# Three chained stages on one core: expert outputs transposed and kept on chip, final MLP run in expert order

## The chip, the cores and the metric

The kernel runs on one core of one Trainium2 chip. The metric is device time in microseconds (us), the median of three runs. One profiled execution of the kernel before is read alongside.

## The reference, cut to what matters

```python
# 1. attention: q, k, v [4, 8, 576, 64]; heads 0-3 see 32 keys back, heads 4-7 every 4th of 128 back
attn = softmax(where(mask, q @ k.T / 8, -1e9));  x = attn @ v          # -> [2304, 512]
# 2. mixture of experts, one of 8 per token
e_idx  = argmax(x @ w_gate)                                            # [2304]
gate_w = softmax(x @ w_gate)[e_idx];  eom = sigmoid(x @ w_output_gate)
out[e_idx == e] = gate_w * eom[:, e] * (relu(x[e_idx == e] @ w1[e]) @ w2[e])   # w1 [8,512,1024], w2 [8,1024,512]
# 3. MLP
result = softplus(out @ w_in) @ w_out                                  # w_in [512,2048], w_out [2048,512]
```

Everything is float32. With the reference's own inputs the eight experts get 370, 280, 356, 312, 196, 203, 278 and 309 tokens.

## The kernel before, in words

All three stages run in one program. TensorE (PE) multiplies float32 data in the fp32r form, each operand split into a high and a low part, so that every product is three matmuls: high by high, low by high, high by low.

**Attention** runs in a loop of two turns of two batches. At its end the token rows are stored to DRAM (`x_tokens`) by the ACT queue, and the gate logits are kept.

**Routing** is one chain of small VectorE (DVE) operations, L950 to L1040, each waiting for the last (`step`). It finds each token's expert and its place in a padded order of slots of 384 rows: slots 0 to 7 belong to experts 0 to 7, and up to five overflow slots take what an expert has over 384. The inverse of that order (`source_i`, which token stands in which row) is made with one-hot matrices: `place_onehot` (a token's place in its block of 128; ACT makes 13 of the 18 token tiles, L777 and L780, DVE the rest) and `block_token` (L999, L1001, with float32 inputs), multiplied in 18 matmuls (L545). At the same time POOL makes the low parts of the first three expert weight chunks (L406).

**Experts.** `Fori(0, E)` over slots. POOL gathers the rows of the next slot with three indirect DMAs (L384), PE transposes them (L554, L562), ACT and DVE split them to `x_hi` and `x_lo`. The hidden size 1024 is cut in eight chunks. For each chunk `f`, `product1` is 12 matmuls whose moving width is the slot's size, and `product2` is 3 matmuls per tile of 128 tokens, 512 columns wide, with the tokens as the stationary side. The slot's size is the smallest of `SIZES = (384, 320, 288, 256)` that holds its tokens (slot 0 always takes 384). PE's program has one unrolled body for each size and picks it by nested `If`s in `sized_slot`. The weights of the next chunks come in a ring of four (`raw`, 512 KB a chunk); ACT writes `w_hi` (L770) and DVE `w_lo` (L1046). The results go over `y_sb` to DRAM (`y_sorted`). Then a loop over the five overflow slots (L642, L643) is walked, whose body (again all four sizes) is jumped over if the slot is not used. Here no slot is.

**Between experts and MLP** all engines meet (`experts_over`), and POOL gathers the first 384 rows from `y_sorted` back in token order (L435). DVE scales them, PE transposes them (L554), ACT and DVE split them.

**MLP.** Six groups of 384 tokens, 16 chunks each: 12 matmuls of 384 columns and 9 of 512. Twelve chunks of weights were split and kept during the experts (`m_hi`, `m_lo`, by POOL), four are split in the first group. The rows of the next group are gathered, scaled and transposed inside each group (12 transposes, L562). Results leave over `y_sb` and the SP queue (L315).

Of the kernel before, what the change touches and what calls it, by code (L numbers as in the profile page):

```python
# [41 lines left out]
SIZES = (SLOT, 320, 288, 256)  # L42
OVER = (N - SLOT) // SLOT
XROWS = (E + OVER) * SLOT
BLOCKS = (E + OVER + 1) * TPS
# [4 lines left out]
RING = 4  # L50
AHEAD = RING - 1
KEPT = FC2 - RING
SCALE = 1.0 / float(np.sqrt(D))
# [5 lines left out]
PLACES_ACT = 13  # L59
# [7 lines left out]
def build(nc, qT, kT, vw, wg, we, wm, out):  # L67
    assert OVER == 5 and NT * P == N and GROUPS * SLOT == N
    ctx = ExitStack()
    with ctx:  # L70
# [8 lines left out]
        ys_d = nc.dram_tensor("y_sorted", (XROWS, DM), F32).ap()  # L79
# [4 lines left out]
        dest_i = sb(ctx, "dest_i", [P, NT], I32)  # L84
        source_i = sb(ctx, "source_i", [P, BLOCKS], I32)
        scale_t = sb(ctx, "scale_t", [P, NT])
        flags_i = sb(ctx, "flags_i", [1, OVER + 1], I32)
        taken_i = sb(ctx, "taken_i", [1, E + OVER], I32)
        raw = sb(ctx, "raw", [P, RING, WCOLS])
        w_hi = sb(ctx, "w_hi", [P, RING, WCOLS], F32R)  # L90
        w_lo = sb(ctx, "w_lo", [P, RING, WCOLS], F32R)

# [5 lines left out]
        v_sb = [sb(early, f"v_sb{s}", [P, UNITS, H, D]) for s in range(2)]  # L98
        x_sb = sb(early, "x_sb", [P, NT, DM])
# [7 lines left out]
        emin8 = sb(early, "emin8", [P, E])  # L107
        thresholds = sb(early, "thresholds", [P, OVER])
        slot_no = sb(early, "slot_no", [P, OVER])
        not_first = sb(early, "not_first", [P, E, NT])  # L110
        column_no = sb(early, "column_no", [P, P])
        block_row = sb(early, "block_row", [P, BLOCKS])
        token_no = sb(early, "token_no", [P, NT])
        logits_01 = sb(early, "logits_01", [P, NT, 2, 2 * E])
        logits_23 = sb(early, "logits_23", [P, NT, 2 * E])
        with ExitStack() as attn:
            probs = sb(attn, "probs", [QT, BANKS, HEADS, KEYS])
# [6 lines left out]
        route = {n: sb(early, f"route_{n}", [P, NT]) for n in  # L124
                 ("m", "first", "sum", "z", "ez", "den", "r", "b1", "b2", "over", "dest", "place", "block")}
# [7 lines left out]
        ov = sb(early, "ov", [P, E])  # L133
        ov_cum = sb(early, "ov_cum", [P, E])
        base2 = sb(early, "base2", [P, E])
        fl = sb(early, "fl", [P, OVER + 1])
        fl_cmp = sb(early, "fl_cmp", [P, OVER, E])
        taken = sb(early, "taken", [P, E + OVER])
        rank_i = sb(early, "rank_i", [P, NT], I32)
        place_onehot = sb(early, "place_onehot", [P, NT, P], F16)  # L140
        in_block = sb(early, "in_block", [P, NT, BLOCKS])
        block_token = sb(early, "block_token", [P, NT, BLOCKS], F16)
# [3 lines left out]

        xs_sb = sb(ctx, "xs_sb", [P, TPS, DM])
        x_hi = sb(ctx, "x_hi", [P, KC, SLOT], F32R)
        x_lo = sb(ctx, "x_lo", [P, KC, SLOT], F32R)
        h_hi = sb(ctx, "h_hi", [P, RING, SLOT], F32R)  # L150
        h_lo = sb(ctx, "h_lo", [P, RING, SLOT], F32R)
        y_sb = sb(ctx, "y_sb", [P, TPS, DM])
        yg_sb = sb(ctx, "yg_sb", [P, TPS, DM])
        soft = sb(ctx, "soft", [P, 2, SLOT])
        g_sb = sb(ctx, "g_sb", [P, 2, SLOT])
        raw_m = sb(ctx, "raw_m", [P, WCOLS])
        m_hi = sb(ctx, "m_hi", [P, KEPT, WCOLS], F32R)
        m_lo = sb(ctx, "m_lo", [P, KEPT, WCOLS], F32R)

# [8 lines left out]
        m_h_ps = [bank[0], bank[1], bank[3]]  # L168
        t_ps = [bank[2], bank[3], bank[7], bank[2]]
        first_t_ps = t_ps[0:3] + [bank[6]]  # L170
# [9 lines left out]
        zero_filled = sem("zero_filled")  # L180
# [8 lines left out]
            exp_in_ready, exps_gate_done, dest_ready, route_done, x_stored, place_ready, place_distances, place_onehots, \  # L189
            block_tokens, sources_summed, sources_ready = map(sem, (  # L190
                "tile_done", "x_copied_act", "x_copied_dve", "route_step",
                "onehot_ready", "ranks_done", "exp_in_ready", "exps_gate_done", "dest_ready", "route_done",
                "x_stored", "place_ready", "place_distances", "place_onehots", "block_tokens", "sources_summed", "sources_ready"))
        raw_loaded = [sem(f"raw_loaded{r}") for r in range(RING)]
        first_rows = [sem(f"first_rows{j}") for j in range(TPS)]
        first_gathered = [sem(f"first_gathered{j}") for j in range(TPS)]
        w_hi_done, w_lo_done = sem("w_hi_done"), sem("w_lo_done")
        rows_loaded, rows_t_done, x_hi_done, x_lo_done = map(sem, (
            "rows_loaded", "rows_t_done", "x_hi_done", "x_lo_done"))
        g1_done, g2_done, h_hi_done, h_lo_done, y_copied, y_stored, y_all_stored = map(sem, (  # L200
            "g1_done", "g2_done", "h_hi_done", "h_lo_done", "y_copied", "y_stored", "y_all_stored"))
        mraw_loaded, m_hi_done, m_lo_done = sem("mraw_loaded"), sem("m_hi_done"), sem("m_lo_done")
        experts_over, overflow_stored = sem("experts_over"), sem("overflow_stored")
        tail_loaded = [sem(f"tail_loaded{r}") for r in range(RING)]
        tail_hi_done, tail_lo_done = sem("tail_hi_done"), sem("tail_lo_done")
        gathered, rows_scaled, m_rows_t_done, m_x_hi_done, m_x_lo_done = map(sem, (
            "gathered", "rows_scaled", "m_rows_t_done", "m_x_hi_done", "m_x_lo_done"))
# [5 lines left out]
        SCORE_CREDIT, PT_CREDIT, OUT_CREDIT, TILE_CREDIT, PLACE_CREDIT, W_CREDIT, H_CREDIT, G_CREDIT, G2_CREDIT, Y_CREDIT = \  # L213
            BANKS, 1, 2, 2, 1, RING, 2, 3, 1, 1
# [937 lines left out]
```

## Time and profile before

| what | value |
|---|---|
| median of 3 runs (lowest, highest) | 855.58 us (854.88, 857.57) |
| profiled execution, span | 854.7 us, 0.9 us under the median |
| PE busy | 788.7 us, 92% |
| DVE busy | 426.5 us, 50% |
| ACT busy | 400.4 us, 47% |
| POOL busy | 142.7 us, 17% |
| attention | 0 to 136.6 us |
| routing, up to the first expert matmul | to 165.2 us |
| experts | to 417.8 us |
| between experts and MLP | to 438.7 us |
| MLP, up to its last copy | to 849.7 us |

Busy time is an average over stages. PE is busy nearly all the time in attention, experts and MLP; it is nearly idle in the routing and between experts and MLP. A matmul's start to start, not its duration, tells its price, since matmuls overlap.

### The profile page before, as it was taken

To read this page: it belongs to the slowest core of one execution; us is meant where nothing else is said; L and a number is where in the kernel's file an instruction comes from. 1 tells how busy PE (TensorE), PEld (TensorE's weight loads), DVE (VectorE), ACT (ScalarE), POOL (GpSimd) and SP (SyncE) were. 2 spreads that over 40 slices of the span, in tenths; PEclk is the share of its full clock that TensorE was granted. 3 is DMA by queue.
4 is the path that set the end of the run, shared out by engine and by line. 5 is a ranking of instruction groups with operands and counts; after the bars stand their busy time and mean duration, and the time that the engine had idled before them with its cause. 6 is when DMAs were issued, how large, how long until landed. Compare 5 with 4: busy or idle time off the path is not lost.

```text
span 854.7 us, 13304 instructions
## 1 busy us (share of the span) xinstructions
PE 788.7 (92%) x4472; PEld 688.2 (81%) x4473; DVE 426.5 (50%) x856; ACT 400.4 (47%) x1015; POOL 142.7 (17%) x139
## 2 busy tenths in 40 slices
PE   5998993498999999999569999999999999999997
PEld 3676673497899998889459999989999999999996
DVE  7886977543644466655134434443434434434332
ACT  4885983333445456544134344334335335335332
POOL 4220223322331332514120100100100100000000
PEclk9999997599999999999859999999999999999999
DMA  9568905245464677754140100100100100000000
GB/s 258 151 186 289 247 5 184 78 144 199 151 219 142 237 258 249 238 201 172 40 173 0 38 23 15 37 0 37 37 0 37 35 2 37 0 0 37 1 1 38
DMA packets 35796, 89.66 MB, mean 105 GB/s; under 512 B 3824, under 2 KB 12016, under 8 KB 35248
## 3 DMA queue, kind: packets, MB, share of 16 engines
q1 hardware_dynamic: 28032, 66.36, 24.1%
q0 software_dynamic: 5328, 18.09, 6.7%
q10 hardware_dynamic: 2400, 4.72, 1.5%
q8 instruction: 23, 0.38, 0.2%
q14 instruction: 13, 0.11, 0.0%
HBM read 69.50 MB, written 19.66 MB: 104 GB/s over the span
## 4 chain that ended last, share of the span: by engine, by line
PE 79%; PEld 6%; DVE 4%; issue 4%; DMA 2%; ACT 2%; PEldq 2%; SPq 1%; POOL 0%; ACTq 0%; DVEq 0%; POOLq 0%
PE bank L573 11%; PE bank L575 11%; PE bank L574 11%; PE bank L584 11%; PE bank L586 11%; PE bank L582 11%; PE bank L460 4%; PE bank L484 2%; PE bank L497 2%; PE bank L470 2%; PE bank L562 1%; DMA v_sb<-vw 1%; PEld bank L573 1%; PEld bank L575 1%; PEld bank L586 1%
## 5 line engine op out<-in xcount | busy, mean ns | idle before, releaser
L1095 DVE SCALAR_TENSOR_TENSOR g_sb<-bank,soft 128x384 f32<-128x384 f32 x96 | 53.6, 558 | 229.4 <-ACT soft L846 229.4
L842 ACT ACTIVATE soft<-bank 128x384 f32<-128x384 f32 x96 | 47.3, 492 | 209.6 <-PE bank L575 209.6
L1046 DVE TENSOR_TENSOR w_lo<-raw,w_hi 128x1024 fp32r<-128x1024 f32 x65 | 89.3, 1373 | 78.8 <-ACT w_hi L770 77.8
L573 PE MATMUL bank<-x_hi,w_hi 128*128 128x384 f32 (+3 forms) x352 | 112.2, 319 | 5.3 <-issue 3.7
L575 PE MATMUL bank<-x_hi,w_lo 128*128 128x384 f32 (+3 forms) x352 | 111.9, 318 | 0.6 <-issue 0.6
L574 PE MATMUL bank<-x_lo,w_hi 128*128 128x384 f32 (+3 forms) x352 | 111.7, 317 | 0.0
L770 ACT ACTIVATE w_hi<-raw 128x1024 fp32r<-128x1024 f32 x68 | 71.8, 1058 | 77.1 <-PE bank L586 75.5
L582 PE MATMUL bank<-w_hi,h_hi 128*128 128x512 f32 x248 | 99.6, 402 | 0.5 <-DVE h_lo L1059 0.5
L573 PE MATMUL bank<-x_hi,m_hi 128*128 128x384 f32 x288 | 98.2, 341 | 0.6 <-DVE x_lo L1053 0.6
L575 PE MATMUL bank<-x_hi,m_lo 128*128 128x384 f32 x288 | 98.1, 341 | 0.0
L574 PE MATMUL bank<-x_lo,m_hi 128*128 128x384 f32 x288 | 97.8, 339 | 0.0
L586 PE MATMUL bank<-w_hi,h_lo 128*128 128x512 f32 x248 | 97.5, 393 | 0.0
L584 PE MATMUL bank<-w_lo,h_hi 128*128 128x512 f32 x248 | 97.4, 393 | 0.0
L586 PE MATMUL bank<-m_hi,h_lo 128*128 128x512 f32 x216 | 85.5, 396 | 0.0
L584 PE MATMUL bank<-m_lo,h_hi 128*128 128x512 f32 x216 | 85.3, 395 | 0.0
L582 PE MATMUL bank<-m_hi,h_hi 128*128 128x512 f32 x216 | 84.0, 389 | 0.0
L710 ACT ACTIVATE probs<-bank,neg_max 96x128 f32<-96x128 f32 x192 | 67.3, 364 | 23.1 <-DVE neg_max L881 23.1
L573 PEld LDWEIGHTS bank<-x_hi,w_hi 128*128 128x128 f32 x352 | 67.4, 192 | 10.2 <-issue 4.6
L574 PEld LDWEIGHTS bank<-x_lo,w_hi 128*128 128x128 f32 x352 | 67.4, 191 | 3.2
L575 PEld LDWEIGHTS bank<-x_hi,w_lo 128*128 128x128 f32 x352 | 67.4, 191 | 0.0
L435 POOL DMA_INDIRECT yg_sb<-y_sorted,dest_i x18 | 18.5, 1029 | 254.8 <-DVE xs_sb L1084 226.3
L573 PEld LDWEIGHTS bank<-x_hi,m_hi 128*128 128x128 f32 x288 | 55.1, 191 | 3.6 <-DVE x_lo L1053 1.0
(147 smaller groups left out, 1347.9 us busy)
## 6 DMA issues: line engine op xcount, KB each, us to landing
raw<-we SPq DMA_DIRECT2D x64, 512.0 KB, 3.9
raw_m<-wm POOLq DMA_DIRECT2D x12, 512.0 KB, 8.1
y_sorted<-y_sb SPq DMA_DIRECT2D x24, 256.0 KB, 5.3
x_tokens<-x_sb ACTq DMA_DIRECT2D x6, 768.0 KB, 5.8
out<-y_sb SPq DMA_DIRECT2D x18, 256.0 KB, 2.1
v_sb<-vw SPq DMA_DIRECT2D x4, 1024.0 KB, 12.0
y_sorted<-k_sb SPq DMA_DIRECT2D x1, 3840.0 KB, 31.0
q_sb<-qT SPq DMA_DIRECT2D x4, 768.0 KB, 8.1
```

Source lines behind the costliest of these rows:

```text
L460: last = nc.tensor.matmul(bank_[0:QT, 2 * KEYS * n_pair:2 * KEYS * (n_pair + 1)], q_sb[b][:, pair, q0:q0 + QT], k_sb[b][:, pair, :, k0:k0 ...
L573: nc.tensor.matmul(bank_[:, 0:rows], hi[:, w], x_hi[:, k, 0:rows], start=(k == 0), stop=False)
L574: nc.tensor.matmul(bank_[:, 0:rows], hi[:, w], x_lo[:, k, 0:rows], start=False, stop=False)
L575: last = nc.tensor.matmul(bank_[:, 0:rows], lo[:, w], x_hi[:, k, 0:rows], start=False, stop=(k == KC - 1))
L582: nc.tensor.matmul(y_ps[j][:, :], h_hi[:, f % RING, c], hi[:, DM:2 * DM], start=(f == 0), stop=False, skip_group_check=True)
L584: nc.tensor.matmul(y_ps[j][:, :], h_hi[:, f % RING, c], lo[:, DM:2 * DM], start=False, stop=False, skip_group_check=True)
L586: last = nc.tensor.matmul(y_ps[j][:, :], h_lo[:, f % RING, c], hi[:, DM:2 * DM], start=False, stop=(f == n_f - 1), skip_group_check=True)
L710: last = nc.scalar.activation(probs[:, c, h, :], s_ps[c][0:QT, KEYS * h:KEYS * (h + 1)], ACT.Exp, bias=neg_max[:, c, h:h + 1], scale=SCALE ...
L770: nc.scalar.activation(w_hi[:, r, :], raw[:, r, :], ACT.Copy).then_inc(done, 1)
L842: nc.scalar.activation(u, m_h_ps[f % 3][:, 0:SLOT], ACT.Abs).then_inc(soft_step, 1)
L1046: nc.vector.tensor_tensor(w_lo[:, r, :], raw[:, r, :], w_hi[:, r, :].bitcast(F32), ALU.subtract).then_inc(done, 1)
L1095: nc.vector.scalar_tensor_tensor(g_sb[:, f % 2, :], m_h_ps[f % 3][:, 0:SLOT], 0.0, soft[:, f % 2, :], ALU.max, ALU.add).then_inc(g_done, 1)
```

## The change

- The experts' `product2` is turned round: the weights are the stationary side and the slot's tokens the moving side, so it is 12 matmuls of the slot's size per chunk instead of 3 matmuls of 512 columns per tile. Its result is y transposed, which is copied (four ACT copies) into `yT_sb`, on chip, at the expert's start column. `y_sorted`, its zero fill, the meeting of the engines, the second gather and the MLP's transposes are gone.
- The MLP walks the tokens in expert order; `group_rows_hi` and `group_rows_lo` split straight from `yT_sb`. The results are scattered to `out` by 18 indirect DMAs on POOL, whose row numbers come from `expert_order`, a DRAM table written by 18 indirect DMAs on POOL ahead of the expert loop.
- Each token's scale is stored to DRAM and gathered by three more indirect DMAs per slot; ACT scales the expert's input rows (`scale_rows`) ahead of their transposes.
- `SIZES` gets a fifth entry, 224, and slot 0 takes its real size; the overflow body is one unrolled size (384).
- The one-hots are all made on DVE from 16-bit inputs. DVE also makes the low parts of the first four weight chunks, which POOL no longer does.
- The ring is eight chunks, four split ahead; `w_lo` is written over `raw`. A chunk is loaded once `g2_done` says its place is free. Eight MLP chunks are kept and eight split in the first group.
- Only two PSUM banks hold transposes, so they are done as (0, 1) and (2, 3), with a wait on `x_lo_done` between.

```diff
-SIZES = (SLOT, 320, 288, 256)
+SIZES = (SLOT, 320, 288, 256, 224)
-RING = 4
-AHEAD = RING - 1
+RING = FC1
+AHEAD = 4
...
+                if not slot:
+                    pool.wait_ge(scales_stored, 16)
+                for j in range(TPS):
+                    c = slot * TPS + j
+                    pool.indirect_dma_start(
+                        out=row_scale[:, c:c + 1], out_offset=None, in_=scale_d,
+                        in_offset=bass.IndirectOffsetOnAxis(ap=source_i[:, c:c + 1], axis=0)
+                        ).then_inc(rows_loaded if slot else first_rows[j], 16)
...
-            for f in range(AHEAD):
-                pool.wait_ge(w_hi_done, f + 1 + W_CREDIT)
-                nc.gpsimd.tensor_tensor(w_lo[:, f, :], raw[:, f, :], w_hi[:, f, :].bitcast(F32), ALU.subtract
-                                        ).then_inc(w_lo_done, 1)
...
+            pool.wait_ge(positions_ready, 1)
+            for t in range(NT):
+                pool.indirect_dma_start(
+                    out=order_d, out_offset=bass.IndirectOffsetOnAxis(ap=position_i[:, t:t + 1], axis=0),
+                    in_=token_ids[:, t:t + 1], in_offset=None).then_inc(order_written, 16)
+            pool.wait_ge(order_written, 16 * NT)
+            pool.dma_start(out_rows_i[:, :], order_d.rearrange("(p t) o -> p (t o)", p=P)).then_inc(out_rows_loaded, 16)
...
+            def product2_columns(f, hi, lo, done, rows):
+                for k in range(KC):
+                    w = slice(DM + P * k, DM + P * (k + 1))
+                    y = yT_ps[k][:, 0:rows]
+                    nc.tensor.matmul(y, hi[:, w], h_hi[:, f % HRING, 0:rows], start=(f == 0), stop=False,
+                                     skip_group_check=True)
+                    nc.tensor.matmul(y, lo[:, w], h_hi[:, f % HRING, 0:rows], start=False, stop=False,
+                                     skip_group_check=True)
+                    last = nc.tensor.matmul(y, hi[:, w], h_lo[:, f % HRING, 0:rows], start=False,
+                                            stop=(f == FC1 - 1), skip_group_check=True)
+                last.then_inc(done, 1)
...
                 for f in range(FC1):
                     p1(f)
+                    if f == FC1 - 1:
+
+                        pe.wait_ge(rows_scaled, slot * TPS + 2 * TPS)
+                        transpose_rows((0, 1))
                     if f:
-                        if f == FC1 - 1:
-
-                            pe.wait_ge(rows_loaded, slot * (16 * TPS) + 16 * TPS)
-                            transpose_rows((0, 1, 2), rows_t_done)
                         p2(f - 1)

-                pe.wait_ge(x_lo_done, slot * KC + (KC + 1))
-                transpose_rows((3,), rows_t_done)
+                pe.wait_ge(x_lo_done, slot * KC + (KC + 2))
+                transpose_rows((2, 3))
                 p2(FC1 - 1)
...
                 with pe.If(n < used):
-                    sized_slot(n + E)
-            pe.drain().then_inc(experts_over, 1)
-            pe.wait_ge(experts_over, 5)
+                    slot_products(n + E, SLOT)
...
+                    if f == FC1 - 2:
+
+                        act.wait_ge(rows_loaded, slot * (32 * TPS) + 32 * TPS)
+                        for j in range(TPS):
+                            scale_rows(slot + 1, j)
...
+            V.tensor_tensor(place_onehot[:, :, :], column_no[:, :, :],
+                            place[:, :].unsqueeze(1).to_broadcast([P, P, NT]), ALU.is_equal).then_inc(block_tokens, 1)
+            step(V.tensor_tensor(in_block[:, :, :], block_row[:, :, :],
+                                 block_of[:, :].unsqueeze(1).to_broadcast([P, BLOCKS, NT]), ALU.is_equal))
```

## Rows read from the trace of the kernel before

**Rows 1.** Busy time by stretch: PE, PEld, DVE, ACT, POOL, then PEclk, DMA share, GB/s

```profile
136.60:165.24 28.64, 4.80 (x33) 2.98 (x33) 21.87 (x60) 10.40 (x23) 10.96 (x7) 0.58 0.33 110
165.24:417.80 252.56, 247.19 (x1392) 221.94 (x1392) 132.21 (x159) 118.50 (x178) 81.25 (x60) 0.99 0.57 191
417.80:438.65 20.85, 3.44 (x13) 2.14 (x13) 2.07 (x5) 2.71 (x7) 4.13 (x5) 0.57 0.31 95
438.65:849.68 411.03, 410.99 (x2076) 372.71 (x2076) 164.36 (x330) 169.14 (x330) 14.39 (x14) 0.99 0.07 24
...
165.24:168.30 3.06, 3.06 (x10) 3.06 (x11) 0.80 (x2) 0.00 (x0) 2.45 (x4) 0.51 0.55 146
```

**Rows 2.** Groups by form: first products of the slots of size 256

```profile
L573 PE MATMUL bank<-x_hi,w_hi 128*128 128x256 f32 x64 | 18.2, 284 | 0.5 <-issue 0.5
```

**Rows 3.** Timeline of PE in slots 2 and 5: start, us, instruction

```profile
240.22 0.33 PE L573 MATMUL bank<-x_hi,w_hi 128*128 128x384 f32 x1
...
242.30 0.39 PE L582 MATMUL bank<-w_hi,h_hi 128*128 128x512 f32 x1
...
244.38 0.33 PE L573 MATMUL bank<-x_hi,w_hi 128*128 128x384 f32 x1
...
330.34 0.28 PE L573 MATMUL bank<-x_hi,w_hi 128*128 128x256 f32 x1
...
332.61 0.28 PE L574 MATMUL bank<-x_lo,w_hi 128*128 128x256 f32 x1
```

**Rows 4.** Timeline of PE: first matmul of slots 1 and 5

```profile
204.94 0.39 PE L573 MATMUL bank<-x_hi,w_hi 128*128 128x288 f32 x1 [3.27 <-issue]
...
329.89 0.38 PE L573 MATMUL bank<-x_hi,w_hi 128*128 128x256 f32 x1 [0.46 <-issue]
```

**Rows 5.** Chain that ended last, between experts and MLP: start, us, what

```profile
419.39 7.81 PEldq L643
...
432.69 3.68 DMA yg_sb<-y_sorted,dest_i
```

**Rows 6.** Instruction DMA: whole span, 0:165, 165:240, 414:438, 438:855 (packets, MB, share)

```profile
q8 instruction: 23, 0.38, 0.2%
...
q8 instruction: 4, 0.07, 0.2%
...
q8 instruction: 8, 0.13, 0.7%
...
q8 instruction: 5, 0.08, 2.0%
...
q8 instruction: 6, 0.10, 0.1%
```

**Rows 7.** Timeline of DVE in the routing

```profile
137.94 0.31 DVE L955 TENSOR_TENSOR routee_d<-logits,route_m 128x144 f32<-128x144 f32 x1
...
138.97 2.01 DVE L959 TENSOR_TENSOR onehot_b<-emin,route_first 128x144 bf16<-128x144 f32 x1
...
143.38 2.33 DVE L963 TENSOR_TENSOR routee_tmp<-logits,routee_onehot 128x144 f32<-128x144 f32 x1
...
152.66 0.94 DVE L1001 TENSOR_TENSOR block_token<-in_block,token_no 128x756 f16<-128x756 f32 x1
...
155.53 0.19 DVE L1011 CAST source_i<-source 128x42 int32<-128x42 f32 x1
```

**Rows 8.** Timeline of POOL: weight splits and a row gather

```profile
138.44 7.10 POOL L406 TENSOR_TENSOR w_lo<-raw,w_hi 128x1024 fp32r<-128x1024 f32 x3 [13.69 <-ACT w_hi L770]
...
159.37 0.95 POOL L384 DMA_INDIRECT xs_sb<-x_tokens,source_i  x1 [0.30 <-issue]
```

**Rows 9.** Timeline of ACT at the end of the program

```profile
849.68 1.57 ACT L853 ACTIVATE y_sb<-bank 128x512 f32<-128x512 f32 x3 [4.56 <-PE bank L586]
```

**Rows 10.** Chain that ended last: transposes at the end of an MLP group

```profile
504.45 0.98 PE bank L562 x9
```

**Rows 11.** Groups by line: split of a weight chunk on DVE

```profile
L1046 DVE TENSOR_TENSOR w_lo<-raw,w_hi 128x1024 fp32r<-128x1024 f32 x65 | 89.3, 1373 | 78.8 <-ACT w_hi L770 77.8 <-issue 1.0
```

More of the change, by code:

```diff
@@ L97, in build @@
         k_sb = [sb(early, f"k_sb{s}", [P, PAIRS, 2, S]) for s in range(2)]
-        v_sb = [sb(early, f"v_sb{s}", [P, UNITS, H, D]) for s in range(2)]
-        x_sb = sb(early, "x_sb", [P, NT, DM])
+        x_sb = sb(early, "x_sb", [P, TILES_TURN, DM])
         xT_sb = sb(early, "xT_sb", [P, KC, 2 * S])
@@ L116, in build @@
         with ExitStack() as attn:
+            v_sb = [sb(attn, f"v_sb{s}", [P, UNITS, H, D]) for s in range(2)]
             probs = sb(attn, "probs", [QT, BANKS, HEADS, KEYS])
@@ L124, in build @@
         route = {n: sb(early, f"route_{n}", [P, NT]) for n in
-                 ("m", "first", "sum", "z", "ez", "den", "r", "b1", "b2", "over", "dest", "place", "block")}
+                 ("m", "first", "sum", "z", "ez", "den", "dest", "shift", "position", "index")}
         routee = {n: sb(early, f"routee_{n}", [P, NT, E]) for n in
@@ L142, in build @@
-        block_token = sb(early, "block_token", [P, NT, BLOCKS], F16)
+        per_expert = {n: sb(early, f"expert_{n}", [P, E]) for n in
+                      ("ov", "ov_cum", "before", "row", "counted", "shift", "limit", "end")}
+        per_slot = {n: sb(early, f"slot_{n}", [P, SLOTS]) for n in ("expert", "expert8", "start", "taken")}
+        slot_cmp = sb(early, "slot_cmp", [P, SLOTS, E])
+        slot_tmp = sb(early, "slot_tmp", [P, SLOTS, E])
+        place_i = sb(early, "place_i", [P, NT], I32)
@@ L666, in p2 @@
                     pe.wait_ge(g_lo_done, g * FC2 + (f + 1))
-                    product2(f, FC2, *chunk(f), m_g2_done)
+                    product2_rows(f, *chunk(f), m_g2_done)
                 for f in range(FC2):
@@ L863, in _ @@
         def _(dve):
+            for n in range(2):
+                nc.vector.memset(bank[n][:, 2 * TW:SLOT], 0.0)
             for s in range(2):
@@ new lines, in _ @@
+            step(V.tensor_tensor(X["end"][:, :], count, X["row"][:, :], ALU.add))
+            step(V.tensor_tensor(slot_tmp[:, :, :], slot_cmp[:, :, :], over_slots(X["end"][:, :]), ALU.mult))
+            step(V.reduce_sum(SL["taken"][:, :], slot_tmp[:, :, :], axis=AX.X))
+            step(V.scalar_tensor_tensor(SL["taken"][:, :], slot_no[:, :], float(-SLOT), SL["taken"][:, :],
+                                        ALU.mult, ALU.add))
+            step(V.tensor_scalar(SL["taken"][:, :], SL["taken"][:, :], 0.0, None, ALU.max))
@@ new lines, in _ @@
+            step(V.tensor_copy(used_i[:, :], X["ov_cum"][0:1, E - 1:E]))
+            step(V.tensor_copy(expert_i[:, :], SL["expert"][0:1, :]))
+            step(V.tensor_copy(start_i[:, :], SL["start"][0:1, :]))
+            V.tensor_copy(taken_i[:, :], SL["taken"][0:1, :]).then_inc(route_done, 1)
+            step(V.tensor_tensor(RE["tmp"][:, :, :], RE["onehot"][:, :, :], over_t(X["shift"][:, :]), ALU.mult))
+            step(V.reduce_sum(R["shift"][:, :], RE["tmp"][:, :, :], axis=AX.X))
+            step(V.tensor_tensor(R["position"][:, :], R["dest"][:, :], R["shift"][:, :], ALU.add))
```

502 lines of the change are left out of this document (229 added, 273 removed).

## The prediction

> **What bounds the kernel now.** I read the page first: PE is busy 92% of the span, so only PE's work and PE's idle stretches can move the end. Then I cut the span into stages [rows 1]. In experts and MLP PE is busy for 247.2 of 252.6 us and for 411.0 of 411.0. In the routing it works 4.8 of 28.6 us, and between experts and MLP 3.4 of 20.9. So there are two kinds of gain: fewer matmul columns, and shorter gaps. The reader should see that DVE, ACT and POOL have room in the experts (132, 119 and 81 of 253 us), and that DMA is at 57% there.
>
> The price of a matmul is its start to start. In slot 2, 12 matmuls of 384 columns take 2.08 us and 9 of 512 take 2.08; in slot 5, 19 of 256 take 2.27 [rows 3]. That is 0.173, 0.231 and 0.120 us, or 0.00042 us per column; between them 320 columns cost 0.146 and 288 cost 0.133, and continued, 224 cost 0.106.
>
> The sizes: 256 columns occur 64 times in one of the three forms of `product1`, that is two slots of 32 [rows 2]; 320 and 288 likewise two each, 384 the other two. The token counts give 384, 288, 384, 320, 256, 256, 288, 320, and after the change 224 for slots 4 and 5.
>
> **The matmuls of the experts.** `product2` per chunk goes from 9 x 0.231 = 2.08 (6 x 0.231 = 1.39 at size 256) to 12 times the slot's price: 384: 2.08, no gain; 320: 1.75, so 0.33 x 16 chunks = 5.2 us; 288: 1.60, 0.48 x 16 = 7.7; 224: 1.27, 0.12 x 16 = 1.9. `product1` at 224 saves 12 x 0.0135 x 16 = 2.6. Together -17.3. If 224 columns are no quicker than 256, `product2` there costs 1.43 and the gain is 12; those are the ends.
>
> **The routing.** Three DVE operations with 144 elements take from 138.97 to 145.71 us, 6.7 us, while a fourth of the same size takes 0.31 [rows 7]. They stand under POOL's three weight splits, which run from 138.44 to 145.54 [rows 8]. Without those splits they cost about 3 x 0.34. The rest of the new chain to `source_i`: 15 small operations, 4.2 us by their neighbours; three one-hot operations of 2304, 756 and 756 elements, 2.6 + 0.9 + 0.9 = 4.4 by the 0.94 us row with float32 inputs; PE's 18 small matmuls and two conversions, 1.5. From 138.9 that makes 11.6 us against 16.8 now (to 155.72): -5.2, between -3 and -7.5 (half the price for the 16-bit operations is the lower end; I take the row). The Trainium skill, page "VectorE: DVE Perf Modes", section "Mode 2×_1P", says that two-source operations on 16-bit contiguous data give two results per cycle; no row here shows it, and by it the routing would be another 2 us shorter.
>
> From `source_i` to the first product are 9.5 us now. Three more gathers follow the row gathers on POOL, at 1.3 us each (0.95 and 0.30 of issue [rows 8]); the last starts 6.8 us after `source_i` and lands 3.6 later (a gather on its way takes 3.68 [rows 5]). Then ACT's scaling 0.6 and the 2.2 us that follow a landing today. That is 13.2. DVE arrives at the same time: 21 slot operations, eight position operations, a register load and four splits of 1.23 to 1.37 us [rows 11]. +3.8, between +2.5 and +6.
>
> **Slot 0 waits for slot 1's rows.** POOL's queue now has, before `load_rows(1)`, 18 scatters at 1.3 us, the wait for their landing, a load and a register load; six gathers follow. From `source_i`: 8 + 23.4 + 3 + 1.5 + 6.5, last landing +3.6: 45.5. PE wants the scaled rows after the last `product1` of slot 0, at 13.3 + 1.4 (low clock) + 29.2 = 43.9; ACT needs 1.6 for scaling. So PE stalls 3.2, and the late ACT and DVE work costs about 1.3 more: +4.5, from 0 (gathers of single words quicker) to +7.
>
> **Slot changes.** Before the second transpose pair PE waits for two `x_lo` instead of one, and ACT has the row scaling (1.5 us) and a weight split (1.0) in front of the last `h_hi`. At size 224 a `product` lasts 1.3 us; ACT and DVE reach `x_lo` 1 about 1.15 us late, at 288 about 0.25; two slots each, +2.9 (0 to +6). PE's own branch code shows as "issue": 0.46 us before slot 5 [rows 4]. The 224 body lies one `If` deeper (0.4 us) and the last product is shorter, so three changes show 1 to 1.5 us instead of two with 0.6: +2.0 (1 to 4).
>
> **Code that is not loaded.** Slot 1 starts after 3.27 us of "issue" [rows 4], when PE for the first time jumps over three bodies; the first jumps over the overflow body hold PE's queue for 7.81 us [rows 5]. Instruction blocks of 16 KB explain it: eight come from 165 to 240 us, and as 4 + 8 + 5 + 6 make all 23, none from 240 to 414, where six slots run on what is held [rows 6]. After the change a body has 204 matmuls instead of 180, and there are five: matmuls and their weight loads go from 1392 to 2040. The bodies of 288 and 224 now lie behind ones that never ran, so each first entry should miss once: 3.7 us at slot 1 and 3.7 plus the clock's fall at slot 4. I take +9; from 0 (held or fetched early) to +36 (the first rival).
>
> **Between experts and MLP.** The gap is 20.85 us now [rows 1]. After: four copies of y (1.6), ACT's walk over the overflow loop, x_hi 0.5, x_lo 0.55: 4.4. PE's queue walks the same loop, some 5 us, starting 2 us before the array ends, plus 0 to 3.7 for a jump over a body that is a quarter as long. I take 6.9: -14, from -6.5 (the 7.8 us jump stays) to -17. The low clock at the start remains: ten matmuls in 3.06 us at 0.51 [rows 1].
>
> **MLP and end.** Five groups lose 12 transposes, 9 of which take 0.98 [rows 10]: 1.3 x 5 = -6.5. The splits of `x_hi`, `x_lo` lie under the last two `product2`. At the end ACT's copies start at 849.68 [rows 9] and today all is over at 854.7. POOL's three scatters would start at 850.4, 851.8 and 853.1 and land 3.6 later, and 0.8 follows, as today: 857.5, +2.8 (1.5 to 4). The stores inside the MLP are hidden by a whole group of 68 us.
>
> **Sum.** -17.3 - 5.2 + 3.8 + 4.5 + 2.9 + 2.0 + 9 - 14 - 6.5 + 2.8 = -18.0 against the span of 854.7: 836.7, and the median stands 0.9 higher: 838. Attention keeps its operations; the raw loads move to a time when DMA waits for nobody.
>
> **Rivals.** First, on the other side: the five bodies don't stay loaded. Then each change of slot meets one or two blocks that are gone, 3.7 us each with little cover, and the clock falls after each: over six changes some 5 to 6 us each, +27 over my +9: 865. For it speak the 47% more code and the price of a jump to code that is not held; against it, that 174 us passed without one load [rows 6]. It decides from about 18 us more than my sum. The Trainium skill, page "Runtime: NRT & Kernel Launch", section "Instruction fetch mechanics", gives PE room for 2048 instructions and a stall for a taken branch outside what is held; by it 1392 and a few would fit, as the trace shows, and 2040 and a few would not, which is this rival.
>
> Second: the chain of small waits is worse than I add up. POOL's 18 scatters take 2 us each, ACT becomes late in every slot, the 224 slots run at ACT's and DVE's pace: +12, 850.
>
> Third: the code is held and the overflow jump is short, -9 and -3: 826.
>
> **Chances.** My case 0.45, the first rival 0.25, the second 0.15, the third 0.15. A measurement of this kernel tells about 0.3% (2.6 us) from no change. Faster takes my case, the third and most of the second, and a little of the first: 0.72; same 0.05; slower 0.23. The range 824 to 868 leaves 0.1 on either side. My own case alone spans 829 to 847.
>
> **What would show it.** Right: in the routing, the three 144-element operations at 0.3 us each; PE's "issue" only at slots 1, 4 and 5; slots of 320 near 28 us and of 288 near 26; 5 to 8 us before the MLP; MLP groups of 66.8 us. A wait of PE for scaled rows at the end of slot 0 near 3 us. Wrong: instruction packets spread over all slots, "issue" of 3 us or more at most slot changes, `product2` at 224 columns no quicker than 0.12 us a matmul, or an overflow jump that still holds PE for 12 us.

## The result and the profile after

The changed kernel takes **919.18 us** (median of 4 runs, 916.03 to 919.76), the kernel before 855.23 (852.80 to 857.57): ratio 1.0737, 95% interval 1.0712 to 1.0762. It is 7.4% slower. The forecast was 838 us with a range of 824 to 868 and "faster" at 0.72: wrong in sign and outside the range. The time given below for the kernel called four_both is the median of its three fast executions (828.3 to 829.3 us); its other three took 843.9 to 848.3, and its trace is of the one at 848.3, so that trace can't be set beside this time.

The page of the changed kernel: first the span, then busy time per engine, the clock in 40 slices (tenths of full speed), the instruction DMA (packets, MB, share), the chain, and the costliest group of instructions.

```profile
span 914.3 us, 13460 instructions
...
PE 776.8 (85%) x4640; PEld 701.0 (77%) x4641; DVE 419.5 (46%) x854; ACT 409.5 (45%) x1041; POOL 164.7 (18%) x172
...
PEclk9999995977999978697888999999999999999997
...
q8 instruction: 48, 0.79, 0.4%
...
PE 75%; issue 11%; DVE 5%; POOL 4%; ACT 3%; DMA 0%; ACTq 0%; POOLq 0%; DVEq 0%
...
L557 PE MATMUL bank<-x_hi,w_hi 128*128 128x384 f32 (+3 forms) x448 | 149.8, 334 | 71.0 <-issue 69.9
```

PE waits 69.9 us for nothing that the profile names ("issue"), all of it ahead of one kind of instruction, the first product of a slot, where the kernel before had 3.7. And 48 blocks of instructions are fetched where it was 23 [rows 6].

Busy time by stretch: routing from the same point as before, experts, gap, MLP, end. Two short rows behind them show the products after a stall.

```profile
136.60:159.86 23.26, 5.43 (x33) 3.76 (x33) 20.11 (x66) 6.76 (x12) 9.79 (x8) 0.50 0.17 52
159.86:490.86 331.00, 246.36 (x1632) 243.09 (x1632) 127.55 (x159) 127.14 (x208) 99.81 (x90) 0.86 0.40 133
490.86:495.88 5.02, 0.17 (x3) 0.00 (x1) 0.62 (x2) 2.81 (x7) 0.00 (x0) 0.83 0.40 134
495.88:899.65 403.77, 403.73 (x2016) 366.17 (x2016) 161.50 (x319) 172.43 (x333) 14.52 (x15) 0.99 0.03 10
899.65:914.30 14.65, 0.00 (x0) 0.00 (x0) 0.00 (x0) 1.57 (x3) 2.88 (x3) 0.64 0.14 54
...
328.50:333.75 5.25, 5.25 (x24) 5.25 (x25) 1.41 (x2) 1.44 (x2) 3.40 (x2) 0.50 0.01 3
```

Set against [rows 1] this is the whole account: up to the first product -5.4 us (165.24 to 159.86), experts +78.4 (252.56 to 331.00), gap -15.8 (20.85 to 5.02), MLP -7.3 (411.03 to 403.77), end +9.6 (5.0 to 14.65). The sum is +59.6, the difference of the spans. Everything but the experts and the end went about as forecast. The prediction's signs of being wrong came true: 40 of the 48 instruction packets come in the expert stage, at nearly every slot, and "issue" of 3 us or more at most slot changes. In the experts PE is busy for 246 of 331 us, at a mean clock of 0.86 where it was 0.99.

The timeline of PE, first transpose at the end of slot 0 and first product of slots 1, 2, 4, 5, 6 and 7, with the idle time before each and what ended it:

```profile
199.90 1.54 PE L546 MATMUL bank<-ident,xs_sb 128*128 128x128 f32 x6 [9.14 <-ACT xs_sb L766]
...
216.32 0.60 PE L557 MATMUL bank<-x_hi,w_hi 128*128 128x288 f32 x1 [8.77 <-issue]
...
249.98 0.68 PE L557 MATMUL bank<-x_hi,w_hi 128*128 128x384 f32 x1 [3.79 <-issue]
...
328.50 0.55 PE L557 MATMUL bank<-x_hi,w_hi 128*128 128x224 f32 x1 [9.56 <-issue]
...
377.41 0.55 PE L557 MATMUL bank<-x_hi,w_hi 128*128 128x224 f32 x1 [21.85 <-issue]
...
418.18 0.60 PE L557 MATMUL bank<-x_hi,w_hi 128*128 128x288 f32 x1 [14.24 <-issue]
...
459.52 0.63 PE L557 MATMUL bank<-x_hi,w_hi 128*128 128x320 f32 x1 [11.69 <-issue]
```

Six of seven slot changes stall. Slots 4 and 5 are of the same size and run the same body, and still the change between them is the longest. In the trace's records of PE's sequencer these stalls are branches: a jump takes 0.07 to 0.35 us when all is well, and in the expert stage 15 of them take 2.7 to 6.1 us, 70.9 us together. Ahead of slot 5 they stand in a row (start, us, line):

```
353.62 3.58 L635   end of the loop, back to its start
358.03 5.32 L628   past the body of 384
363.54 5.69 L628   past the body of 320
369.50 2.74 L628   past the body of 288
372.42 4.50 L628   past the body of 256
```

And after these stalls PE starts at the lower of its two clock levels (0.50 granted, 1.2 GHz). After the one of 9.56 us, 24 products of 224 columns took 5.25 us at 0.50 (row 328.50 above), 0.22 us each, where later ones take 0.112; after the one of 3.79 us too, products of 384 columns start 0.32 us apart where later ones start 0.173 apart.

### The profile page after: what moved, and what is told of

It is laid out like the page before. It is cut to its first block, busy times and chain, and to the rows that moved or that the text cites. A ratio compares the mean times of both kernels' runs of the same rounds, so it can differ in the third digit from the quotient of the medians.

```text
span 914.3 us, 13460 instructions
## 1 busy us (share of the span) xinstructions
PE 776.8 (85%) x4640; PEld 701.0 (77%) x4641; DVE 419.5 (46%) x854; ACT 409.5 (45%) x1041; POOL 164.7 (18%) x172
## 4 chain that ended last, share of the span: by engine, by line
PE 75%; issue 11%; DVE 5%; POOL 4%; ACT 3%; DMA 0%; ACTq 0%; POOLq 0%; DVEq 0%
PE bank L557 11%; PE bank L559 11%; PE bank L558 11%; PE bank L580 7%; PE bank L582 7%; PE bank L578 7%; PE bank L445 3%; PE bank L567 3%; PE bank L571 3%; PE bank L569 3%; POOL expert_order L396 2%; PE bank L469 2%; PE bank L482 2%; PE bank L455 2%; PE bank L546 1%
## 5 line engine op out<-in xcount | busy, mean ns | idle before, releaser
L557 PE MATMUL bank<-x_hi,w_hi 128*128 128x384 f32 (+3 forms) x448 | 149.8, 334 | 71.0 <-issue 69.9
L558 PE MATMUL bank<-x_lo,w_hi 128*128 128x384 f32 (+3 forms) x448 | 148.2, 331 | 0.0
L559 PE MATMUL bank<-x_hi,w_lo 128*128 128x384 f32 (+3 forms) x448 | 148.1, 331 | 0.0
L557 PEld LDWEIGHTS bank<-x_hi,w_hi 128*128 128x128 f32 x448 | 90.3, 202 | 74.9 <-issue 71.3
L1059 DVE SCALAR_TENSOR_TENSOR h_lo<-bank,h_hi 128x384 fp32r<-128x384 f32 x64 | 35.6, 557 | 156.8 <-ACT h_hi L783 151.5
L567 PE MATMUL bank<-h_hi,w_hi 128*128 128x384 f32 (+3 forms) x256 | 79.7, 311 | 1.6 <-issue 1.6
L569 PE MATMUL bank<-h_hi,w_lo 128*128 128x384 f32 (+3 forms) x256 | 78.1, 305 | 0.0
L571 PE MATMUL bank<-h_lo,w_hi 128*128 128x384 f32 (+3 forms) x256 | 78.0, 305 | 0.0
L557 PE MATMUL bank<-x_hi,m_hi 128*128 128x384 f32 x192 | 65.7, 342 | 4.9 <-DVE x_lo L1084 4.9
L559 PE MATMUL bank<-x_hi,m_lo 128*128 128x384 f32 x192 | 65.6, 341 | 0.0
L558 PE MATMUL bank<-x_lo,m_hi 128*128 128x384 f32 x192 | 65.3, 340 | 0.0
```

The lines of the kernel that those rows point to most:

```text
L557: nc.tensor.matmul(bank_[:, 0:rows], hi[:, w], x_hi[:, k, 0:rows], start=(k == 0), stop=False)
L558: nc.tensor.matmul(bank_[:, 0:rows], hi[:, w], x_lo[:, k, 0:rows], start=False, stop=False)
L559: last = nc.tensor.matmul(bank_[:, 0:rows], lo[:, w], x_hi[:, k, 0:rows], start=False, stop=(k == KC - 1))
L567: nc.tensor.matmul(y, hi[:, w], h_hi[:, f % HRING, 0:rows], start=(f == 0), stop=False, skip_group_check=True)
L569: nc.tensor.matmul(y, lo[:, w], h_hi[:, f % HRING, 0:rows], start=False, stop=False, skip_group_check=True)
L571: last = nc.tensor.matmul(y, hi[:, w], h_lo[:, f % HRING, 0:rows], start=False, stop=(f == FC1 - 1), skip_group_check=True)
```

## The experiments

All ratios are to the kernel before, timed beside each. Instructions are counted in the built programs; a block is the 16 KB of one instruction fetch, 256 instructions. A slow jump is a branch record of PE's sequencer of 2.7 us or more; "in the loop" leaves out those over the overflow body behind it.

**First four: one body less, two bodies less, and never-run bodies added to the kernel before.**

```diff
 a_no256: -SIZES = (SLOT, 320, 288, 256, 224)
          +SIZES = (SLOT, 320, 288, 224)
 a_three: +SIZES = (SLOT, 320, 224)
 b_dose1 (kernel before), b_dose2 with it twice:
                 from_size(0)
+                with pe.If(taken > N):
+                    slot_products(slot, SLOT)
```

> The changed kernel without the 256-row body. No expert of this input takes it (the loads are 370, 280, 356, 312, 196, 203, 278, 309 rows), so every product that runs is the same; the tensor engine's expert loop is 437 instructions shorter (1,751 in place of 2,188; the kernel before has 1,515). Theory A (the bodies of the expert loop no longer stay loaded): the 15 jumps of 2.7 to 6.1 us, 71 us in all, mostly vanish, and the time is 848 to 865; the instruction packets fall from 48 to under 32. If only some vanish, between 865 and 900. Rival B (the longer chain of branches and value loads costs in itself): only experts 4 and 5 pass one branch less, 1 to 2 us together, so 916 to 919. Rival C (low clock and late rows set the gaps): no change, 919.

> The changed kernel with bodies for 384, 320 and 224 rows alone: 1,314 instructions in the loop, fewer than before. Two experts of 280 and 278 rows now take 320 rows in place of 288: 2 x 192 products x (0.147 - 0.133) us = 5.4 us more. Theory A: no jump over 2 us is left; 916 - 71 + 5.4 plus what the clock gives back (up to 17): 835 to 853. Rival B: 919 + 5.4 - 3 = 921. Rival C: 924.

> The kernel before with one more 384-row body at the end of the expert loop that no expert ever takes (its condition is more rows than there are tokens). The work is unchanged; the loop grows from 1,515 instructions to about 1,900. Theory A, form 1 (what counts is the length of the loop, blocks that are only jumped over too): some stalls, 858 to 890. Theory A, form 2 (only blocks that run count): one more jump per expert that lands in one more block, 855 to 860. Rival B: 8 branches more at 0.3 to 0.5 us, 858.

> The kernel before with two more such bodies that no expert takes: the loop has about 2,290 instructions, more than the changed kernel's 2,188. Theory A, form 1: stalls as in the changed kernel, 15 or more of 3 to 6 us, 890 to 930. Theory A, form 2: two more blocks for the two landings, 856 to 870. Rival B: 16 branches more at 0.3 to 0.5 us, 861.

Measured: a_no256 921.02 us (1.0751, 1.0707 to 1.0796), a_three 864.93 (1.0085, 1.0051 to 1.0119), b_dose1 856.0 (0.9991) and b_dose2 857.4 (1.0005). The last two say nothing of the question: the build knows that `taken` can't pass N and left the bodies out, so these are 21 more executions of the kernel before (their traces show the same 61 branches of PE as its own). The other two are the finding. Taking out 437 of 2,188 instructions of the loop gave nothing: 14 slow jumps remain, and theory A's 848 to 865 was missed by 56 us. Taking out the same again removed 56 us and all slow jumps in the loop but two, though theory A had expected none and 835 to 853. So stalls do not grow evenly with the code, they set in at a limit. Rivals B (branch depth) and C (late rows), which a_no256 alone could not rule out, are out: they expected 921 to 924 for a_three.

A rule that fits, made after these runs: PE holds eight blocks, beside the running block it always takes in the next one, and the one unused for longest goes. Worked through over the paths of the eight experts it gives 1 slow jump in the loop for the kernel before (1 seen), 15 for the changed kernel (15), 13 for a_no256 (14), 1 for a_three (2). The loops touch 7, 10, 8 and 6 blocks. It makes two odd predictions, and the next runs test them.

**Same code, moved by 109 instructions; and a never-run body that the build can't leave out.**

```diff
 a_aligned: SIZES = (SLOT, 320, 288, 224), and
+            for _ in range(218):
+                pe.wait_ge(block_tokens, 2)
             first_transposes()
 b_extra (kernel before):
                 from_size(0)
+                with pe.If(used > 3):
+                    slot_products(slot, SLOT)
```

(The build folds two waits into one instruction.)

> The changed kernel without its 256-row body, with 109 more instructions (waits that are already met) on the tensor engine before the first transposes. The expert loop keeps its 1,751 instructions but now lies in seven pieces of 256 instructions in place of eight. Theory A1 (the engine keeps eight such pieces and always takes the next one beside the one that it runs, the longest unused goes): with that rule the run without the 256-row body should show 13 slow jumps (14 were seen), the one with three bodies 1 (2 were seen), the changed kernel 15 (15 were seen); here it gives 2. So the slow jumps fall from 14 to 2 to 4, and the time from 921 to 850 to 862. Rival A2 (the number of instructions or of bodies counts, not where they lie): 14 slow jumps, 921 to 927. Rival C (late rows, clock): 921 to 927.

> The kernel before with one more 384-row body at the end of the expert loop, under a condition that this input never meets but that the build can't decide (more than three overflow slots); in the two runs with the other condition the build had left the bodies out, so they were repeats of the kernel before. The work is unchanged, the loop has about 1,905 instructions, in nine pieces of 256 of which eight are run or landed in. Theory A1: 21 slow jumps in place of 1, at 3.6 to 6 us each of which the queue in front of the engine hides up to 1: 925 to 960. Rival A2 (only what is executed counts): 8 more branches, 857 to 862. Rival B (bodies that are never run are harmless as the repeats seemed to say): 856.

Measured: a_aligned **871.84** (1.0177, 1.0138 to 1.0217), 49 us faster than a_no256 with more instructions in the program and not one less in the loop; 5 slow jumps in the loop instead of 14. Of the 49 us, 41 are PE's idle time ahead of the slots' first products (64.5 us in a_no256, 23.8 here). The rest can't be split: it holds the low clock behind the stalls, and a_no256 ran on another chip, where a few `h_hi` copies came late (below). b_extra **969.14** (1.132, 1.1285 to 1.1354), 113 us slower than the kernel before although every product is the same and the added body never runs; 24 slow jumps in the loop. The rule had 2 and 21, so it is right in kind and a little mild, and both times lie above what theory A1 expected (850 to 862, 925 to 960). A2 ("only what is executed counts", or "the number of instructions counts") is out by 49 and over 100 us. Instruction DMA (packets, MB, share) in the expert stage of the changed kernel, 160 to 491 us, and of b_extra, 165 to 534 us:

```profile
q8 instruction: 40, 0.66, 0.9%
```

```profile
q8 instruction: 59, 0.97, 1.4%
```

The kernel before has 8 from 165 to 240 us and none from there to 414 [rows 6]. The timeline of PE in b_extra, ahead of slot 4:

```profile
350.45 0.58 PE L573 MATMUL bank<-x_hi,w_hi 128*128 128x256 f32 x1 [26.75 <-issue]
```

**The scatters, and the end of the program.** The base is a_three, whose stages are quiet enough to see these.

```diff
 three_moved:
-            for t in range(NT): ...scatter t of expert_order...   (ahead of load_rows(1))
             for s in range(E):
                 slot_rows(s)
                 keep_mlp_chunk(s)
+                if s < 6: order(3 * s, 3 * s + 3)
+                if s == 6: ...wait for all, load out_rows_i...
 three_ends:
                 pool.wait_ge(out_stored, (g + 1) * (16 * TPS))
                 pool.sem_inc(out_place_free, 1)
+                if g < GROUPS - 1:
+                    pool.drain()
 and around the overflow loop on PE
+            with pe.If(used > 0):
                 with pe.Fori(0, OVER) as n:
 three_drain: only the drains.  three_lastbut: one drain, at g == GROUPS - 2
```

> The changed kernel with bodies for 384, 320 and 224 rows, and the 18 scatters of the expert order moved on GpSimd from before the rows of expert 1 to three behind each of the experts 0 to 5, the load of the order behind expert 6. Theory S (the scatters hold up the row gathers of expert 1 and so the transposes at the end of expert 0): the waits of 3.5 and 0.9 us at L546 around 198 to 206 go, and with them part of the low clock behind them: 3 to 7 us less than the 865 of the kernel with three bodies, 858 to 862. Rival T (the wait only moves: the scatters now hold up a later expert's rows or the MLP chunks): 865 or more.

> The changed kernel with bodies for 384, 320 and 224 rows; the overflow loop stands under one condition (any overflow slot at all), and GpSimd drains behind the scatters of each of the first five groups. Ends: the drain of GpSimd after the last scatter took 8.16 us in the changed kernel and is the last thing of the program. If it works off what has gathered since the last drain, it now takes 2 to 4 us and the end is 4 to 6 us earlier; if it has a price of its own, 8 us again and nothing is gained. Into the MLP: two slow jumps over the overflow body, 4.66 and 6.78 us, and a gap of 13.5 us in the three-body kernel; under one condition one of them is left, and the gap falls by 5 to 7 us. Together 852 to 860 in place of 865.

> Three bodies and the drains of GpSimd behind the scatters of the first five groups, without the one condition around the overflow loop. The last drain took 8.16 us in the three-body kernel and 0.28 us in the run with both edits. In the three-body kernel the scalar engine also began 14 of 64 h_hi copies 1.3 to 6.2 us after the product that they need, for no cause that the profile names, and in the run with both edits one. If those late copies are chance of the build, this run has few of them: 865 - 8 - 14 = 843. If they come with the plain overflow loop: 857.

three_moved 842.47 (0.9842, 0.9814 to 0.9870), three_ends 835.61 (0.9760, 0.9729 to 0.9790), three_drain 845.30 (0.9877, 0.9836 to 0.9917). The first two are faster than their edits explain against a_three's 864.93, below the ranges of 858 to 862 and 852 to 860. For three_drain I took off 8 us for the drain and 14 for late copies (843). So a_three itself was run again, and one more placing of the drain with it:

> The three-body kernel once more, unchanged. If the late h_hi copies belong to the build: 861 to 869 again, and 10 or more late copies in the trace. If they were chance of that chip or that load: 850 to 856, with few or none.

> The three-body kernel with one drain of GpSimd, behind the scatters of the last group but one. If a drain works off what the indirect transfers have left since the last one, this drain takes about 7 us while the tensor engine works, the one at the end 0.28 us, and the time is 8 us under that of the plain three-body kernel. If late copies come from chance, few or none: 842 to 848.

three_again **852.73** (0.9967, 0.9942 to 0.9992), 12 us less than the same kernel on another chip; three_lastbut 845.41 (0.9885, 0.9824 to 0.9946). What differs in the traces is one kind of wait, that of ACT for the products (total us, times, longest). First a_three, then three_again:

```profile
ACT h_hi L783 <- PE bank L559: 100.7, 49, 5.8
ACT h_hi L783 <- remote: 20.4, 7, 5.8
```

```profile
ACT h_hi L783 <- PE bank L559: 101.9, 54, 4.8
```

In a_three 14 of the 64 `h_hi` copies began 1.3 to about 6 us after their product; in three_again one did, and that one waits for the scales. They also occur, some six of them, in a_no256, on the same chip, and, 1.7 to 3.4 us late, three times in the changed kernel. What makes them late stays open. The two kernels have the same source, so it isn't the code alone. With 852.7 as the base (ten executions from 847.8 to 855.9) the rest adds up, and the ratios to the kernel before give the same within 1 us, though the runs are of three chips: the drain alone gives 7.4 (three_drain) and 7.3 (three_lastbut), the drain with the condition 17.1, the moved scatters 10.3; all three together make 825.3, and three_both below has 826.4.

The drain (GpSimd's own records): in the changed kernel, the last one runs from 905.87 to 914.03, 8.16 us, and nothing comes after it. With drains in between, the first takes 6.93 us (three_drain, under the MLP) or 7.91 (three_lastbut), and each one after that 0.28, the last one too. How long one takes goes with the number of DMAs that GpSimd has issued since the drain before it, counted in the traces: 3.25 us behind 39 (the kernel before, at 425.56), 6.93 behind 84 (three_ends), 7.91 behind 96, 8.16 behind 99, and 0.28 behind 3. The four long ones lie on one line, 0.07 us and 0.082 for each DMA. So a drain works off what has gathered, as one of the two readings in the expectation for three_ends had it, and it can be taken early under other work. The last drain of the kernel before (7.38 us from 678.08, under the MLP) doesn't belong on the line: three gathers still run inside it.

The condition: three-body kernels have two slow jumps over the overflow body before the MLP (4.66 and 6.78 us in a_three) and a gap of 13.1 to 14.1 us there; with it one jump and 5.01.

**All three edits, with three, four and five bodies.** four_both has the 218 waits too.

> Three bodies, the scatters of the order behind the experts, the drains, and the overflow loop under one condition. The run with drains and condition took 835.6 and still had a wait of 7.26 us at the end of expert 0, for the scales that come behind the 18 scatters. Theory S: that wait goes and the clock behind it stays up: 824 to 830. Rival T (the wait only moves): 833 to 837.

> The same edits with bodies for 384, 320, 288 and 224 rows, lying in seven pieces of 256 instructions as in the run that took 871.8. The last drain gives back 8 us, the condition around the overflow loop 5 to 8, the moved scatters 5 to 9: 847 to 854. Against three bodies it saves 5.4 us of products and pays five slow jumps in place of two, 3 x 4.8 = 14 us and their low clock, so it should stay 15 to 25 us above the three-body version.

> The changed kernel with its five bodies, and the same edits to scatters, drain and overflow loop. It tells what is left when only the code of the expert loop is too long. Theory A: 15 slow jumps or more as before, and 919.2 - 8 (drain) - 9 (wait at the end of expert 0) = 898 to 905. Rival: if the slow jumps were in part waits for GpSimd's queue of scatters, below 885.

three_both **826.36** (0.9657, 0.9635 to 0.9679), four_both 828.9 (0.9688, 0.9668 to 0.9707), five_both 905.28 (1.0584, 1.0564 to 1.0603). three_both came in its expected range and five_both at the top of its own, with 17 slow jumps in the loop where the changed kernel had 15. Four and five bodies run exactly the same products, since no expert takes 256 rows: the 76 us between them come with code that has to be fetched again, and nothing else differs but the 109 instructions of met waits. five_both stands 79 us above three_both, which runs 5.4 us more of products: 84 us for 17 slow jumps in place of 2.

My expectation for four_both (847 to 854) was too high by some 20 us, and the reason stays open. Its trace, of the execution at 848.3, has five slow jumps in the loop and 22.9 us of idle time ahead of the slots' first products, against 5.9 in three_both; its MLP is as quick (403.0 and 403.7 us). How many slow jumps an execution of 828.9 us has, no trace shows, so no price of a jump can be read from it. The same step without the edits to the ends, a_aligned against three_again, costs 871.8 - 852.7 + 5.4 = 24.5 us for three slow jumps more, of which some 3 us are that the padded kernels reach their first product later (163.0 and 163.7 us, against 159.8 in three_again).

three_both, by stretch: experts, gap.

```profile
158.00:408.94 250.94, 240.88 (x1636) 237.74 (x1634) 132.18 (x162) 128.62 (x212) 112.86 (x91) 0.98 0.52 173
408.94:413.95 5.01, 0.31 (x3) 0.04 (x1) 0.47 (x1) 2.66 (x7) 0.00 (x0) 0.85 0.44 146
```

And its page, busy time per engine:

```profile
PE 770.7 (93%) x4640; PEld 695.3 (84%) x4641; DVE 422.2 (51%) x854; ACT 409.3 (50%) x1041; POOL 174.0 (21%) x172
```

The clock in the experts is back at 0.98. This kernel beats the one before by 3.4% and the changed one by 10%.

## Why the prediction was wrong

**The step that failed: "Code that is not loaded", +9 us ("from 0 to +36").** The mechanism stood there, and its rival said outright that the five bodies might not stay loaded. Both prices were far too low. The term measures 84 us between three_both and five_both at equal products. In the changed kernel's own trace it is some 78: PE's "issue" time ahead of the slots' first products is 66 us more than before (69.9 against 3.7), and products at the low clock cost some 12 more. Three things were missed.
- I took each change of slot to meet "one or two blocks that are gone". But the chain of `If`s jumps from body to body through the whole loop, so once the start of the loop is gone, every step of the chain lands in a block that is gone, and each fetch begins only when the one before has ended: five in a row, 21.85 us, between two slots of the same body. One expensive choice of path, not one expensive jump. The five records in a row show the chain; that each lands in a block that is gone is the rule's reading of them.
- I reckoned with 3.7 us for a miss; the 15 took 4.7 us in the mean (70.9 / 15).
- The clock. After every stall of this length PE runs at 0.50 for some microseconds. Summed over the experts, from start to start, products took 20 us more than at their usual price, against 8 in the kernel before; part of the 20 stands behind the stall at the end of slot 0.

What spoke for it was in the rows: the fetches of [rows 6] with the size of the bodies gave 7 blocks held and 10 needed. "174 us passed without one load" is true of 7 and says nothing of 10. The Trainium skill, page "Runtime: NRT & Kernel Launch", section "Instruction fetch mechanics", gives PE 2048 instructions, refilled in blocks of 256, and a stall for a taken branch whose target is outside "the current 2-page window". The traces fit the size: the rule that counts the jumps best holds eight blocks of 256. They don't fit a window of two pages for PE, since six slots over seven blocks ran without one load (240 to 414 us, [rows 6]); the prediction had put it as "outside what is held". They also show that counting instructions against it is not enough. 1,751 instructions stall 14 times when they touch eight blocks and 5 times when they touch seven, and a body that is only jumped over costs 113 us over eight passes. I gave that rival 0.25 and should have given it most.

**The other terms**, in the order of the sum:
- Matmuls of the experts, -17.3 with 0.106 us for 224 columns. Measured 0.111 to 0.113, so 2.3 us less gain (384 products by 0.006); 384 columns 0.173, 320 0.147, 288 0.133, as read.
- Routing, -5.2. Its parts add up to 11.1 us and not the 11.6 written, so -5.7. Measured -8.7 to `source_i`, but 1.9 of that came before the routing: attention ended earlier, and the first routing operation starts at 134.70 us where it was 136.62. The chain itself went from 19.1 to 12.3 us, -6.8, inside my -3 to -7.5. What was mis-sized are the one-hots in 16-bit, 2.5 us for my 4.4. The DVE timeline of the changed kernel:

```profile
137.04 0.31 DVE L951 TENSOR_TENSOR onehot_b<-emin,route_first 128x144 bf16<-128x144 f32 x1
137.26 0.30 DVE L954 TENSOR_TENSOR routee_onehot<-emin,route_first 128x144 f32<-128x144 f32 x1
137.60 0.31 DVE L955 TENSOR_TENSOR routee_tmp<-logits,routee_onehot 128x144 f32<-128x144 f32 x1
...
142.40 1.36 DVE L985 TENSOR_TENSOR place_onehot<-column_no,place 128x2304 f16<-128x2304 f16 x1
143.68 0.55 DVE L987 TENSOR_TENSOR in_block<-block_row,block_of 128x756 f16<-128x756 f16 x1
...
146.80 0.19 DVE L1002 CAST source_i<-source 128x42 int32<-128x42 f32 x1
```

  The three operations of 2.0 to 2.3 us in [rows 7] are at 0.3 now that POOL's splits are gone: that was right. 1.36 us for 2304 elements and 0.55 for 756 make 1,911 elements per us; with float32 inputs 756 took 0.94 [rows 7]. The Trainium skill, page "VectorE: DVE Perf Modes", section "Mode 2×_1P", gives two results per cycle for such operations. Its routing of another 2 us less, the one-hots at half my price, was nearer than my sum: for this term the 32-bit row was the wrong one to lean on.
- `source_i` to first product, +3.8. Measured 12.87 against 9.5: +3.4. Right.
- Slot 0 waits for slot 1's rows, +4.5 with PE stalled 3.2. Measured 9.14 us of stall. The place was right and the size off (the queue's terms add up to 46.0 and not the 45.5 written, which makes the forecast stall 3.7). Eleven of the 18 scatters take 0.97 us and seven 1.30 to 2.04, so from the first to the end of the last it is 27.3 us for my 23.4; the wait for them was 3.8, and `row_scale` came last. GpSimd and ACT in the changed kernel:

```profile
155.85 2.04 POOL L396 DMA_INDIRECT expert_order<-token_ids,position_i  x1 [0.30 <-issue]
...
182.16 0.97 POOL L396 DMA_INDIRECT expert_order<-token_ids,position_i  x1 [0.30 <-issue]
186.96 0.59 POOL L400 DMA_DIRECT2D out_rows_i<-expert_order  x1 [3.83 <-DMA expert_order<-token_ids,position_i]
188.49 1.01 POOL L363 DMA_INDIRECT xs_sb<-x_tokens,source_i  x1 [0.94 <-issue]
...
197.90 1.95 ACT L766 ACTIVATE xs_sb<-xs_sb,row_scale 128x512 f32<-128x512 f32 x3 [10.78 <-DMA row_scale<-token_scales,source_i]
```

  Moving the scatters gave 10.3 us; it takes away the stall, 7.1 us in three_again, and the low clock behind it.
- Slot changes, `x_lo` +2.9: waits of 0.78, 1.51, 1.51 and 0.79 us, 4.6, at the two sizes and with the order foretold. Branch depth +2.0: can't be seen beside the misses in the changed kernel. In the three-body kernels changes without a miss show no idle time over 0.4 us at L557.
- Experts to MLP, -14. Measured -15.8: the jump over the overflow body cost nothing in the changed kernel (its branch took 0.35 us), presumably because the wandering in the loop had fetched its blocks; no run tests that. In a_three it was back with 13.5 us of gap.
- MLP -6.5: measured -7.3. Right.
- End, +2.8 ("1.5 to 4"). Measured +9.6. The three scatters start at 900.5, 901.8 and 903.1 and have landed by 905.8, as I had it; I did not see the drain behind them, because in the kernel before the same drain lies under the MLP on an engine that had nothing left to do. Last row of GpSimd in the changed kernel's timeline, against a span end of 914.3:

```profile
903.05 0.96 POOL L419 DMA_INDIRECT out<-y_sb,out_rows_i  x1 [0.30 <-issue]
```

With the changed kernel's own 78 us for code and 9.6 for the end, my sum would have given 838 - 9 + 78 - 2.8 + 9.6 = 914. The other misses (stall +5.9, `x_lo` +1.7, columns +2.3, against routing -3.5, gap -1.8 and MLP -0.8) bring it to 918, where 919 was measured: the rest of the working holds to a few us. Of the second rival (small waits), the stall and `x_lo` came true, 7.6 us together. The third, 826 with all the code held, is also what three_both took, but that is luck: three_both has the edits to the scatters, the drain and the overflow loop besides, and without them the code nearly all held (three_again) took 852.7.

## What to carry to other kernels

Unrolled bodies inside a loop have a budget on PE. In these kernels it is counted in blocks touched, landings of skipped jumps included (and the next block too, by the rule), not in instructions that run. Before adding a size to such a chain, count the blocks from the start of the loop to its end. Near the limit a small step decides: here the first body less gave nothing and the second 56 us, and a shift of the start by 109 instructions 49 us, where all the saved columns of the experts were worth 15. And when GpSimd's last work moves to the end of the program, count the DMAs that it has issued since its last drain: an early drain, under other work, can pay for them (7.4 us here).

## What the runs showed of the hardware

- A slow jump of PE takes 2.7 to 6.1 us in the changed kernel, up to 7.9 in b_extra. The seven blocks of the kernel before stay in the loop for six slots without a load; with the ten of the changed kernel 40 loads come in the expert stage. An `If` around a body that never runs cost 113 us over eight passes, 14 a pass, where a slot that runs 384 rows takes about 35.
- The next block is taken in beside the running one, by all these counts; this is a rule that fits six kernels, not a thing that a row shows. Its misses in a_aligned (5 seen, 2 foretold), and the 17 slow jumps of five_both beside the 15 of the changed kernel, whose loop has the same bodies, show that something in it is still wrong or missing.
- A drain of GpSimd took 0.082 us for each DMA that it had issued since the drain before: 3.25 us behind 39, 6.93 behind 84, 7.91 behind 96, 8.16 behind 99; behind 3 it took 0.28.
- The same kernel (a_three, three_again) took 864.9 and 852.7 us on two chips, with `h_hi` copies on ACT up to 6 us late in the one and on time in the other. Even the ratio to the kernel before on the same chip moved with it, from 1.0085 to 0.9967.
